# Gate weights held still, block means sent earlier, and the scale of 1/8 moved into the queries

## The chip, the cores and the metric

The kernel runs on one core of a Trainium2 chip. The metric is the device time of one execution in microseconds; several executions are timed and their median counts. A core has five engines with queues of their own: TensorE (PE in the profile, its weight loads PEld), VectorE (DVE), ScalarE (ACT), GpSimd (POOL) and SyncE (SP), which here only issues DMAs. They meet at semaphores.

## The reference, cut to what matters

Three stages follow one another: a banded attention with block summaries, then two mixture-of-experts layers. The change lies in the attention and in the router product that follows it.

```
# q, k, v: 4 batches, 8 heads, 768 rows, 64 columns
k_sum = k.reshape(B, H, 24, 32, D).max(axis=3)
v_sum = v.reshape(B, H, 24, 32, D).mean(axis=3)
scores_l = scale * q @ k.T, kept where |i - j| < 16, else -1e9      # scale = 1/8
scores_s = scale * q @ k_sum.T + log(32)
a = softmax over [scores_l, scores_s]
out = a @ [v, v_sum]                      # becomes x: 3072 tokens of 512
logits = x @ w_gate                       # 3072 x 8; tokens go to experts by these
```

## The kernel before

The attention works on units: a unit is one batch and one pair of heads, so that the 128 partitions hold 2 x 64 head columns. There are 16 units, four to a batch (`HP = 4`). A unit has 12 windows of 64 queries, and a window sees 96 keys and the 24 block summaries, 120 columns (`KW`). Four windows make a group (`GW = 4`), three groups a unit (`NG = 3`), 48 groups in all (`GROUPS`). Everything is in fp32 but the mask.

For a group `n`: `scores(n)` puts the mask and log(32) into a PSUM bank with one bf16 product (L1181) and adds four products of queries and keys (L1184). VectorE takes the maxima of the rows (`maxima`, L818 and L821), ScalarE the exponentials with their sums (`exps`, L652), VectorE the reciprocals (`recip`, L825 and L827), GpSimd multiplies (`normalize`, L472), TensorE transposes the probabilities (`probs_T`, L1193), VectorE copies them to SBUF (`evac_pT`, L833), TensorE multiplies them with the values (`times_v`, L1206, 16 passes), and ScalarE copies the output into `xT` (`evac_o`, L661).

The order on each engine is written out by hand as a loop over n. TensorE does in iteration n: `scores(n + 3)`, `times_v(n - 1)`, `probs_T(n)`, and, where n % 3 is 2, `logits` of the unit before (L1220). VectorE does `recip(n + 1)`, `maxima(n + 3)`, `evac_pT(n)`; where n % 3 is 0 also the maxima of the key blocks two units ahead (L791), where it is 2 a quarter of the value block sums of the next batch (`block_means`, L810, the last quarter also L813). ScalarE does `exps(n + 2)`, `evac_o(n - 1)`, and where n % 3 is 2 it issues the DMA that copies a unit's block means beside its value windows (`load_block_means`, L290, "vw<-vs" in the profile). That DMA waits for the means (`vs_ready`); `times_v` of a unit's first group waits for it. GpSimd does `normalize(n + 1)`, the key windows of a later unit (L458, L460; n % 3 is 0), its queries (L466, L467; n % 3 is 1), and constants for the later stages (n % 3 is 2; the longest block of them at n = 26). The queries of units 0 and 1 are spread by ScalarE (L666).

The router's logits are accumulated over the four units of a batch in one PSUM bank: six products per unit, one for each 128 tokens, with the tokens' columns of `xT` as the weights and the gate weights streamed, padded to 128 columns. VectorE copies a batch's 48 columns to `LM` (`logits_in`, L837). When the last batch's are there, VectorE starts the search that assigns tokens to experts.

The second layer's router has another form already (L1463): `wg2` with 32 columns as the weights, a tile of tokens streamed, and the three tiles of a phase written to partitions 0, 32 and 64 of one bank. ScalarE copies them out (L737) and a transpose turns them (L1467).

```
for c in range(KC):
    for j in range(CT):
        ins = mm(LP[32 * j:32 * j + 32, 0:128], wg2[:, c, :], yT[:, j, c, :], start=(c == 0), stop=(c == KC - 1))
```

Of the kernel before, what the change touches and what calls it, by code (L numbers as in the profile page):

```python
# [5 lines left out]
def banded_attention_two_moe_layers(nc, qT, kT, vwin, vblk, g1, w1a, w2a, skip2, g2, w1b, w2b, out):  # L6
    fp32, bf16, i32 = mybir.dt.float32, mybir.dt.bfloat16, mybir.dt.int32
    ALU = mybir.AluOpType
    ACT = mybir.ActivationFunctionType
# [16 lines left out]
    GW = 4  # L26
# [2 lines left out]
    NB = 3  # L29
    NP = 4  # L30
    SCALE = 1.0 / 8.0
    MASKED = -7985954816.0
    LOG_BLOCK = (27.75, -0.024169921875, 5.7220458984375e-05)
    NT = N // 128
    TB = S // 128
    KC = DM // 128
# [23 lines left out]
    with ctx:  # L60
        def sb(name, shape, dt=fp32):
            return ctx.enter_context(nc.sbuf_tensor(name, shape, dt))
# [19 lines left out]
        revE = sb("revE", [128, E])  # L82
        iotaS = sb("iotaS", [128, NSLOT])
        cnt128 = sb("cnt128", [128, NT])
        wg1 = sb("wg1", [128, KC, WIDE + E * (TB - 1)])
        wg2 = sb("wg2", [128, KC, 32])
        l2T = sb("l2T", [CT * 32, 128])

# [51 lines left out]
        def sba(name, shape, dt=fp32):  # L140
# [70 lines left out]
        bank = [ctx.enter_context(nc.psum_tensor(f"bank{i}", [128, 512], fp32)) for i in range(8)]  # L211

        SC, PT, OB, LG = bank[0:3], bank[3:5], bank[5:7], bank[7]
        LGP = LG[:, 0:TB * E]

        XB, HB, YB, SM, LP = bank[0:2], bank[2:4], bank[4:6], bank[6], bank[7]
        VTP, CNT, TAU = SM[:, 0:256], SM[:, 256:256 + WIDE], SM[:, 384:384 + WIDE]
# [5 lines left out]


        names = """q_in0 q_in1 q_in2 k_in0 k_in1 k_in2 v_in0 v_in1 v_in2 vb_in0 vb_in1 vb_in2 vb_in3 wg1_in const_in ident_ready zeros_ready pads_ready
            band_ready const_ready ksum_ready kw_ready kw_first qz_ready vb_sum vs_ready score_mm max_raw max_ready exp_done
            recip_ready norm_done sum_eps gaps_ready prob_tr prob_evac pv_done o_evac xr_tr xr_evac x_st0 x_st1 x_st2 x_st3
            logit_mm logit_in v_ready v_tr cnt_ready cnt_mm tau_diag tau_mm expert_ready expert_read rows_ready base_mm slot_ready
            onehot_ready blk_ready id_mm idp_ready ids_ready tok_c
            xg_in xg_tr xgT_ready w_in0 w_in1 w2_in0 w2_in1 h_mm h_act y_mm y_evac y_tr yT_ready l2_mm l2T_ready l2_tr l2_evac y_out y_st y_written  # L230
            gate_sub gate_exp rows8_ready base8_mm teA_ready onehot2_ready id2_mm gid2_ready route2_ready
# [62 lines left out]
        def own_part(spread_q, j):  # L294

            return spread_q[D * j:D * j + D, :, QW * j:QW * j + QW]

        def queries_of(q, j):

            return q[D * j:D * j + D, :].rearrange("d (w q) -> d w q", q=QW)  # L300
# [129 lines left out]
        def _(pool):  # L430
# [31 lines left out]
            def queries(u):  # L462
                i = u % NB
                pool.wait_ge(s[f"q_in{i}"], 16 * (u // NB + 1))
                pool.wait_ge(s["score_mm"], NG * (u - 1))
                o.step(g.tensor_copy(own_part(qz[u % 2], 0), queries_of(qc[i], 0)))  # L466
                g.tensor_copy(own_part(qz[u % 2], 1), queries_of(qc[i], 1)).then_inc(s["qz_ready"], 1)  # L467
                pool.wait_ge(s["qz_ready"], u + 1)

            def normalize(n):  # L470
# [169 lines left out]
        def _(act):  # L640
# [6 lines left out]
            def exps(n):  # L647
                act.wait_ge(s["max_ready"], n + 1)
                if n >= NP:
                    act.wait_ge(s["prob_tr"], n - NP + 1)  # L650
                for w in range(GW):
                    ins = a.activation(pr[:, n % NP, w, :], SC[n % 3][:, KW * w:KW * w + KW], ACT.Exp, scale=SCALE,  # L652
                                       bias=nmx[:, n % NP, w:w + 1], accum_out=rsum[:, n % NP, w:w + 1])
                ins.then_inc(s["exp_done"], 1)

            def evac_o(n):
                act.wait_ge(s["pv_done"], n + 1)
                u, gr = divmod(n, NG)
                b, hp = divmod(u, HP)
                at = S * b + GW * QW * gr  # L660
                a.activation(xT[:, hp, at:at + GW * QW], OB[n % 2][:, 0:GW * QW], ACT.Copy).then_inc(s["o_evac"], 1)  # L661

            for u in range(2):
                act.wait_ge(s[f"q_in{u}"], 16)
                for j in range(2):
                    ins = a.activation(own_part(qz[u], j), queries_of(qc[u], j), ACT.Copy)  # L666
                ins.then_inc(s["qz_ready"], 1)
                exps(u)
            for n in range(GROUPS):
                if n + 2 < GROUPS:  # L670
                    exps(n + 2)
                if n >= 1:
                    evac_o(n - 1)
                if n % NG == NG - 1 and 2 <= n // NG + 1 < U:
                    load_block_means(act, n // NG + 1)
            evac_o(GROUPS - 1)

            for t in range(NT):
                act.wait_ge(s["xr_tr"], t + 1)
# [93 lines left out]
        def _(dve):  # L773
# [40 lines left out]

            def maxima(n):
                dve.wait_ge(s["score_mm"], n + 1)
                raw = SC[n % 3][:, GW * KW:GW * KW + GW]
                ve.tensor_reduce(raw, SC[n % 3][:, 0:GW * KW].rearrange("p (w c) -> p w c", w=GW), X, ALU.max,  # L818
                                 negate=True).then_inc(s["max_raw"], 1)
                dve.wait_ge(s["max_raw"], n + 1)  # L820
                ve.tensor_scalar(nmx[:, n % NP, :], raw, SCALE, None, ALU.mult).then_inc(s["max_ready"], 1)  # L821

            def recip(n):
                dve.wait_ge(s["exp_done"], n + 1)
# [8 lines left out]
                ve.tensor_copy(pT[:, n % 2, :], PT[n % 2][0:KW, :]).then_inc(s["prob_evac"], 1)  # L833

            def logits_in(b):
                dve.wait_ge(s["logit_mm"], b + 1)
                ve.tensor_copy(LM[:, TB * b:TB * b + TB, :], LGP.rearrange("p (t e) -> p t e", e=E)) \  # L837
                    .then_inc(s["logit_in"], 1)

            ve.memset(wg1[:, :, :], 0.0)  # L840
            ve.memset(wg2[:, :, :], 0.0).then_inc(s["pads_ready"], 1)
# [11 lines left out]
            for n in range(GROUPS):  # L853
                if n + 1 < GROUPS:
                    recip(n + 1)
                if n + 3 < GROUPS:
                    maxima(n + 3)
                evac_pT(n)
                if n % NG == 0 and n // NG + 2 < U:
                    block_maxima(n // NG + 2)  # L860
                if n % NG == 2 and n // (NG * HP) + 1 < B:
                    block_means(n // (NG * HP) + 1, n // NG % HP)
                if n >= NG * HP and n % (NG * HP) == 2:
                    logits_in(n // (NG * HP) - 1)
            logits_in(B - 1)
            dve.wait_ge(s["logit_in"], B)
# [299 lines left out]
        def _(pe):  # L1166
# [43 lines left out]
            def logits(u):  # L1210
                b, hp = divmod(u, HP)
                if u == 0:
                    pe.wait_ge(s["wg1_in"], 16)
                pe.wait_ge(s["o_evac"], NG * (u + 1))
                if hp == 0 and b >= 1:
                    pe.wait_ge(s["logit_in"], b)
                for t in range(TB):
                    cover = hp == 0 and t == 0
                    wide = WIDE + E * (TB - 1) if cover else WIDE
                    ins = mm(LG[:, E * t:E * t + wide], xT[:, hp, S * b + 128 * t:S * b + 128 * t + 128], wg1[:, hp, 0:wide],  # L1220
                             start=cover, stop=(hp == HP - 1 and t == TB - 1))
                if hp == HP - 1:
                    ins.then_inc(s["logit_mm"], 1)

            def x_rows_tile(t):
                if t >= 2:
# [11 lines left out]
            for n in range(GROUPS):  # L1238
                if n + 3 < GROUPS:
                    scores(n + 3)  # L1240
                if n >= 1:
                    times_v(n - 1)
                probs_T(n)
                if n >= NG and n % NG == 2:
                    logits(n // NG - 1)
            times_v(GROUPS - 1)
            logits(U - 1)


            HID = KC * FC  # L1250
# [291 lines left out]
```

## Time and profile before

| | |
|---|---|
| median of 3 timed executions | 902.52 us (900.97 to 902.87) |
| the profiled execution | 897.85 us, its span 896.1 us |
| busy over the span | PE 849.3 us (95%), PEld 569.7 (64%), DVE 466.4 (52%), POOL 220.2 (25%), ACT 212.1 (24%) |
| the chain that ended last | PE 79%, DVE 13%, DMA 3%, issue 3%, POOL 2%, ACT 1% |
| TensorE's mean granted clock | 0.987 of full speed |

The span goes from the first instruction to the last. The shares are averages over stages of different kinds, so that they say little of one stage. The profiler's chain goes back from the last instruction, at each step to what released it. Matmuls are pipelined: a matmul's own duration holds its latency, and the distance between starts is what it costs in a row of them.

### The profile page before, as it was taken

Reading aid. Unit: us, or ns where it says so; the run is one execution under the profiler, and the core shown is the slowest. Engines: PE = TensorE matmul, PEld = TensorE weight load, DVE = VectorE, ACT = ScalarE, POOL = GpSimd, SP = SyncE. Lnnn points to the kernel's source line nnn. Section 1 sums busy time; section 2 is a strip of 40 time slices with the busy share of each in tenths; the row PEclk is TensorE's granted clock in tenths of the full one; section 3 lists DMA queues with packets and bytes.
Section 4 is the critical chain, followed back from the end, with each engine's and each line's share of the span. In section 5 each row is a group of like instructions: output and inputs, shape, how many; then the busy total and the mean of one; then the engine's idle time right before and its main releaser. Section 6 shows DMA issues by size and latency. Waiting matters only on the chain.

```text
span 896.1 us, 15627 instructions
## 1 busy us (share of the span) xinstructions
PE 849.3 (95%) x5212; PEld 569.7 (64%) x5212; DVE 466.4 (52%) x2118; ACT 212.1 (24%) x670; POOL 220.2 (25%) x321
## 2 busy tenths in 40 slices
PE   5899999798899999999999999999999999999997
PEld 4789888686345455454545555555777686777775
DVE  8689886677777676767677676070360000000000
ACT  4466565330102121221202121211111110101010
POOL 4678875001030110203021120203012121211111
PEclk8899999899999999999999999999999999999999
DMA  7987752345070523406071522555789988889880
GB/s 218 283 235 214 219 164 49 122 162 198 26 259 36 208 85 116 178 11 259 24 246 48 201 93 104 189 200 195 277 292 318 356 303 315 320 325 328 313 297 16
DMA packets 69271, 174.78 MB, mean 195 GB/s; under 512 B 6064, under 2 KB 10672, under 8 KB 69216
## 3 DMA queue, kind: packets, MB, share of 16 engines
q1 hardware_dynamic: 54600, 143.99, 46.8%
q0 software_dynamic: 6960, 21.69, 7.0%
q10 hardware_dynamic: 7656, 8.36, 2.8%
q8 instruction: 35, 0.57, 0.3%
q14 instruction: 20, 0.16, 0.1%
HBM read 149.19 MB, written 23.59 MB: 193 GB/s over the span
## 4 chain that ended last, share of the span: by engine, by line
PE 79%; DVE 13%; DMA 3%; issue 3%; POOL 2%; ACT 1%; DVEq 0%; POOLq 0%; SPq 0%; ACTq 0%
PE bank L1314 15%; PE bank L1300 15%; PE bank L1424 14%; PE bank L1435 14%; DVE junk L915 4%; PE bank L1184 4%; PE bank L1206 3%; PE bank L1193 3%; PE bank L1220 2%; PE bank L1373 2%; DMA vw<-vs 1%; PE bank L1289 1%; PE bank L1450 1%; PE bank L1413 1%; PE bank L1181 1%
## 5 line engine op out<-in xcount | busy, mean ns | idle before, releaser
L1300 PE MATMUL bank<-xgT,W 128*128 128x384 f32 x512 | 182.3, 497 | 0.6 <-ACT xgT L687 0.6
L1314 PE MATMUL bank<-W,hT 128*128 128x512 f32 x384 | 179.2, 602 | 0.0
L915 DVE TENSOR_SCALAR_CACHE_REDUCE junk<-Vt,cand 128x192 bf16<-128x192 f32 x376 | 136.1, 410 | 4.8
L1424 PEld LDWEIGHTS bank<-x2T,W 128*128 128x128 f32 x1152 | 131.4, 192 | 7.8 <-issue 7.8
L1424 PE MATMUL bank<-x2T,W 128*128 128x128 f32 x1152 | 131.9, 275 | 0.0
L1435 PE MATMUL bank<-W,h2T 128*128 128x512 f32 x288 | 126.7, 593 | 0.4 <-ACT h2T L754 0.4
L1072 DVE SCALAR_TENSOR_TENSOR o<-bank,gate,x 128x512 f32<-128x512 f32 x18 | 13.4, 751 | 211.6 <-PE bank L1435 211.6
L1300 PEld LDWEIGHTS bank<-xgT,W 128*128 128x128 f32 x512 | 89.6, 191 | 50.5 <-issue 5.7
L1314 PEld LDWEIGHTS bank<-W,hT 128*128 128x128 f32 x384 | 66.8, 190 | 58.4 <-issue 56.5
L1435 PEld LDWEIGHTS bank<-W,h2T 128*128 128x128 f32 x288 | 53.3, 190 | 60.9 <-issue 60.9
L652 ACT ACTIVATE pr<-bank,nmx 128x120 f32<-128x120 f32 x192 | 66.7, 363 | 33.5 <-DVE nmx L821 19.1
L754 ACT ACTIVATE h2T<-bank 128x512 f32<-128x512 f32 x36 | 21.4, 597 | 216.9 <-PE bank L1424 216.9
L692 ACT ACTIVATE hT<-bank 128x384 f32<-128x384 f32 x64 | 31.4, 490 | 141.5 <-PE bank L1300 141.5
L1184 PEld LDWEIGHTS bank<-kw,qz 128*128 128x128 f32 x384 | 55.9, 209 | 1.7
L1184 PE MATMUL bank<-kw,qz 128*128 128x120 f32 x384 | 55.4, 292 | 0.0
L472 POOL TENSOR_TENSOR pr<-pr,rinv 128x480 f32<-128x480 f32 x48 | 47.3, 985 | 30.5 <-DVE rinv L827 28.7
L281 POOL TENSOR_TENSOR hot_id<-hot,pnum 128x384 bf16<-128x384 f32 x7 | 8.2, 1167 | 179.6 <-DVE hot L979 179.6
L596 POOL COPY now_s<-sidx 128x1 int32 (+1 forms) x18 | 3.3, 183 | 193.3 <-DVE o L1072 193.3
L1373 PEld LDWEIGHTS bank<-cnt,same_e 128*128 128x128 bf16 x136 | 13.2, 97 | 57.8 <-DVE junk L915 54.3
L930 DVE TENSOR_SCALAR_CACHE_REDUCE reached<-bank 128x7 f32<-128x7 f32 x120 | 19.9, 166 | 54.2 <-PE bank L1373 54.2
L558 POOL DMA_INDIRECT xg<-x_rows,gidx x24 | 23.6, 984 | 90.6 <-DVE gidx L895 85.7
L565 POOL DMA_INDIRECT out<-yb,tok_i x24 | 23.6, 985 | 85.6 <-ACT yb L696 82.8
(265 smaller groups left out, 1046.1 us busy)
## 6 DMA issues: line engine op xcount, KB each, us to landing
W<-in_moe_w SPq DMA_DIRECT2D x52, 2048.0 KB, 9.0
vw<-in_vwin SPq DMA_DIRECT2D x16, 576.0 KB
qc<-in_qT SPq DMA_DIRECT2D x16, 384.0 KB, 6.5
kc<-in_kT SPq DMA_DIRECT2D x16, 384.0 KB, 7.9
vb<-in_vblk SPq DMA_DIRECT2D x16, 384.0 KB, 6.7
x_rows<-xr SPq DMA_DIRECT2D x24, 256.0 KB, 2.1
y_rows<-yb ACTq DMA_DIRECT2D x24, 256.0 KB, 2.0
vw<-vs ACTq DMA_DIRECT2D x14, 144.0 KB
```

The lines of the kernel that those rows point to most:

```text
L472: g.tensor_tensor(pr[:, n % NP, :, :], pr[:, n % NP, :, :], rinv[:, n % NP, :].unsqueeze(2).to_broadcast([128, GW, KW]), ALU.mult) \
L652: ins = a.activation(pr[:, n % NP, w, :], SC[n % 3][:, KW * w:KW * w + KW], ACT.Exp, scale=SCALE, bias=nmx[:, n % NP, w:w + 1], accum_out= ...
L692: a.activation(hT[:, r, :], HB[r % 2][:, 0:CAP], ACT.Relu).then_inc(s["h_act"], 1)
L915: ins = ve.tensor_scalar(junk[:, c, :], Vt[:, :], cand[:, c:c + 1].bitcast(fp32), 0.0, ALU.is_ge, ALU.add, accum_out=cnt[:, c:c + 1])
L1184: ins = mm(SC[n % 3][:, KW * w:KW * w + KW], qz[u % 2][:, GW * gr + w, :], kw[u % 2][:, GW * gr + w, :], start=False, stop=(w == GW - 1))
L1193: ins = tr(PT[n % 2][0:KW, 128 * w:128 * w + 128], pr[:, n % NP, w, :], ident[:, :])
L1206: ins = mm(OB[n % 2][D * j:D * j + D, QW * w:QW * w + QW], vw[i][:, GW * gr + w, D * j:D * j + D], pT[:, n % 2, 128 * w + QW * j:128 * w + ...
L1300: ins = mm(HB[r % 2][:, 0:CAP], w1[:, c, 128 * r:128 * r + 128], xgT[:, c, :], start=(c == 0), stop=(c == KC - 1))
L1314: ins = mm(YB[j % 2][:, :], hT[:, r, 128 * j:128 * j + 128], w2[:, r, :], start=(r == 0), stop=(r == FC - 1))
L1373: mm(CNT, same_e[:, :], cnt[:, :].unsqueeze(1).to_broadcast([128, WIDE // 8, 8]), start=True, stop=True).then_inc(s["cnt_mm"], 1)
L1424: ins = mm(HB2[h][:, 128 * c:128 * c + 128], W1[:, par, k * F + at:k * F + at + 128], x2T[par][:, k, :], start=(k == 0), stop=(k == KC - 1))
L1435: ins = mm(YB2[par][:, :], h2T[:, f, :], W2[:, par, f * DM:f * DM + DM], start=(f == 0), stop=(f == FC - 1))
```

## The change

- The logits are computed with the gate weights (32 columns, padded with zeros) as the stationary operand and 256 token columns streamed: three products per unit, to partitions 0, 32 and 64. They come out transposed. After a batch's last unit ScalarE copies 96 x 256 values to a new tile `lgT` (`evac_logits`, at n % 12 = 3 of the next batch), TensorE turns them with two transposes (`logit_rows`, n % 12 = 4), and VectorE copies them to `LM` (n % 12 = 4 instead of 2).
- The block means' DMA is issued at n % 3 = 0 instead of n % 3 = 2.
- The four quarters of the block sums are done at n = 2, 5, 7, 8 in the first batch and at n = 1, 2, 4, 7 of twelve in the others, instead of 2, 5, 8, 11.
- The factor 1/8 is applied as the queries are spread (GpSimd's copies become TENSOR_SCALAR; ScalarE's copies get a scale), and the mask and log(32) are stored times 1/8. So the exponential needs no scale, and the maxima are written once, negated, to `nmx`, which is its bias. L821 and the semaphore between the two are gone.

```
-    MASKED = -7985954816.0
-    LOG_BLOCK = (27.75, -0.024169921875, 5.7220458984375e-05)
+    MASKED = -7985954816.0 * SCALE
+    LOG_BLOCK = (27.75 * SCALE, -0.024169921875 * SCALE, 5.7220458984375e-05 * SCALE)
...
-        wg1 = sb("wg1", [128, KC, WIDE + E * (TB - 1)])
+        wg1 = sb("wg1", [128, KC, 32])
+        lgT = sb("lgT", [3 * 32, S // 3])
...
-        LGP = LG[:, 0:TB * E]
+        LGP = LG[:, S // 3:S // 3 + TB * 32]
...
-                o.step(g.tensor_copy(own_part(qz[u % 2], 0), queries_of(qc[i], 0)))
-                g.tensor_copy(own_part(qz[u % 2], 1), queries_of(qc[i], 1)).then_inc(s["qz_ready"], 1)
+                o.step(g.tensor_scalar(own_part(qz[u % 2], 0), queries_of(qc[i], 0), SCALE, None, ALU.mult))
+                g.tensor_scalar(own_part(qz[u % 2], 1), queries_of(qc[i], 1), SCALE, None, ALU.mult).then_inc(s["qz_ready"], 1)
...
-                    ins = a.activation(pr[:, n % NP, w, :], SC[n % 3][:, KW * w:KW * w + KW], ACT.Exp, scale=SCALE,
+                    ins = a.activation(pr[:, n % NP, w, :], SC[n % 3][:, KW * w:KW * w + KW], ACT.Exp,
...
+            def evac_logits(b):
+                act.wait_ge(s["logit_mm"], b + 1)
+                a.activation(lgT[:, :], LG[0:96, 0:S // 3], ACT.Copy).then_inc(s["lgT_ready"], 1)
...
-                if n % NG == NG - 1 and 2 <= n // NG + 1 < U:
+                if n >= NG * HP and n % (NG * HP) == 3:
+                    evac_logits(n // (NG * HP) - 1)
+                if n % NG == 0 and 2 <= n // NG + 1 < U:
                     load_block_means(act, n // NG + 1)
             evac_o(GROUPS - 1)
+            evac_logits(B - 1)
...
-                raw = SC[n % 3][:, GW * KW:GW * KW + GW]
-                ve.tensor_reduce(raw, SC[n % 3][:, 0:GW * KW].rearrange("p (w c) -> p w c", w=GW), X, ALU.max,
-                                 negate=True).then_inc(s["max_raw"], 1)
-                dve.wait_ge(s["max_raw"], n + 1)
-                ve.tensor_scalar(nmx[:, n % NP, :], raw, SCALE, None, ALU.mult).then_inc(s["max_ready"], 1)
+                ve.tensor_reduce(nmx[:, n % NP, :], SC[n % 3][:, 0:GW * KW].rearrange("p (w c) -> p w c", w=GW), X, ALU.max,
+                                 negate=True).then_inc(s["max_ready"], 1)
...
-                dve.wait_ge(s["logit_mm"], b + 1)
-                ve.tensor_copy(LM[:, TB * b:TB * b + TB, :], LGP.rearrange("p (t e) -> p t e", e=E)) \
-                    .then_inc(s["logit_in"], 1)
+                dve.wait_ge(s["logit_tr"], b + 1)
+                ve.tensor_copy(LM[:, TB * b:TB * b + TB, :].rearrange("p (k i) e -> p k i e", k=3),
+                               LGP.rearrange("p (i k e) -> p k i e", k=3, e=32)[:, :, :, 0:E]).then_inc(s["logit_in"], 1)
...
-                if n % NG == 2 and n // (NG * HP) + 1 < B:
-                    block_means(n // (NG * HP) + 1, n // NG % HP)
-                if n >= NG * HP and n % (NG * HP) == 2:
+                b, at = divmod(n, NG * HP)
+                when = (2, 5, 7, 8) if b == 0 else (1, 2, 4, 7)
+                if b + 1 < B and at in when:
+                    block_means(b + 1, when.index(at))
+                if n >= NG * HP and n % (NG * HP) == 4:
                     logits_in(n // (NG * HP) - 1)
...
-                for t in range(TB):
-                    cover = hp == 0 and t == 0
-                    wide = WIDE + E * (TB - 1) if cover else WIDE
-                    ins = mm(LG[:, E * t:E * t + wide], xT[:, hp, S * b + 128 * t:S * b + 128 * t + 128], wg1[:, hp, 0:wide],
-                             start=cover, stop=(hp == HP - 1 and t == TB - 1))
+                for k in range(3):
+                    at = S * b + S // 3 * k
+                    ins = mm(LG[32 * k:32 * k + 32, 0:S // 3], wg1[:, hp, :], xT[:, hp, at:at + S // 3],
+                             start=(hp == 0), stop=(hp == HP - 1))
...
+            def logit_rows(b):
+                pe.wait_ge(s["lgT_ready"], b + 1)
+                for i in range(TB // 3):
+                    ins = tr(LGP[:, 96 * i:96 * i + 96], lgT[:, 128 * i:128 * i + 128], ident[0:96, 0:96])
+                ins.then_inc(s["logit_tr"], 1)
...
+                if n >= NG * HP and n % (NG * HP) == 4:
+                    logit_rows(n // (NG * HP) - 1)
             times_v(GROUPS - 1)
             logits(U - 1)
+            logit_rows(B - 1)
```

## Rows read from the trace of the kernel before

**Rows 1.** The page's 40 slices, of which TensorE's, its clock's and the DMA's.
```profile
PE   5899999798899999999999999999999999999997
...
PEclk8899999899999999999999999999999999999999
DMA  7987752345070523406071522555789988889880
```

**Rows 2.** Timeline at the end of the attention stage.
```profile
159.19 1.60 PE L1220 MATMUL bank<-wg,xT 128*128 128x128 f32 x12 [0.48 <-ACT xT L661]
160.83 0.21 DVE L837 COPY LM<-bank 128x48 f32<-128x48 f32 x1 [3.35 <-PE bank L1220]
```

**Rows 3.** The chain that ended last, from 0 to 62 us: start, us, what.
```profile
37.49 6.82 DMA vw<-vs
...
46.71 0.61 PE bank L1206 x16
47.33 0.58 PE bank L1193 x4
47.91 1.34 PE bank L1220 x12
49.25 0.20 PE bank L1181
49.45 0.89 PE bank L1184 x8
```

**Rows 4.** Stretches: us; busy PE, PEld, DVE, ACT, POOL; PEclk, DMA share, GB/s.
```profile
20.00:40.00 20.00, 16.76 (x157) 15.07 (x157) 13.48 (x32) 9.78 (x51) 12.77 (x19) 0.75 0.98 269
67.50:75.70 8.20, 8.20 (x101) 7.58 (x100) 7.44 (x18) 5.38 (x27) 7.33 (x11) 1.00 0.77 233
75.70:83.90 8.20, 8.20 (x101) 7.58 (x101) 7.41 (x18) 5.38 (x27) 6.77 (x9) 1.00 0.80 229
```

**Rows 5.** Waits from 40 to 160 us: total us, times, longest.
```profile
PE bank L1206 <- DMA vw<-vs: 3.4, 4, 1.6
...
PE bank L1193 <- POOL pr L472: 1.1, 1, 1.1
...
...
PE bank L1206 <- DVE pT L833: 0.8, 1, 0.8
```

**Rows 6.** The chain from 330 to 336 us, the second router's product.
```profile
333.30 1.00 PE bank L1463 x24
```

**Rows 7.** Timeline from 58 to 62 us, ScalarE's DMA issue and who waited.
```profile
58.33 0.79 ACTq L290 DMA_DIRECT2D vw<-vs  x1
...
61.61 0.69 PE L1206 MATMUL bank<-pT,vw 120*64 120x64 f32 x16 [0.77 <-DMA vw<-vs]
```

**Rows 8.** Timeline from 87 to 89.3 us, VectorE and GpSimd.
```profile
87.21 0.64 DVE L818 TENSOR_REDUCE bank<-bank 128x4 f32<-128x480 f32 x1
...
87.88 0.16 DVE L821 TENSOR_SCALAR nmx<-bank 128x4 f32<-128x4 f32 x1
87.96 0.69 DVE L833 COPY pT<-bank 120x512 f32<-120x512 f32 x1
...
88.38 0.82 POOL L466 COPY qz<-qc 64x768 f32<-64x768 f32 x1
...
88.56 0.66 DVE L825 TENSOR_SCALAR rsum<-rsum 128x4 f32<-128x4 f32 x1
```

**Rows 9.** Groups of instructions, 0 to 185 us.
```profile
L472 POOL TENSOR_TENSOR pr<-pr,rinv 128x480 f32<-128x480 f32 x48 | 47.3, 985 | 30.5 <-DVE rinv L827 28.7 <-PE bank L1184 0.4
...
L810 DVE TENSOR_REDUCE vs<-vb 96x32 f32<-96x1024 f32 x16 | 19.2, 1204 | 1.2 <-DMA vb<-in_vblk 1.2
...
L661 ACT ACTIVATE xT<-bank 128x256 f32<-128x256 f32 x48 | 18.5, 385 | 32.3 <-PE bank L1206 32.2
...
L466 POOL COPY qz<-qc 64x768 f32<-64x768 f32 x14 | 11.4, 817 | 0.0
...
L506 POOL TENSOR_SCALAR iota_blk<-iota_blk 128x24 f32<-128x24 f32 x1 | 0.3, 288 | 0.1
```

More of the change, by code:

```diff
@@ L225, in banded_attention_two_moe_layers @@
         names = """q_in0 q_in1 q_in2 k_in0 k_in1 k_in2 v_in0 v_in1 v_in2 vb_in0 vb_in1 vb_in2 vb_in3 wg1_in const_in ident_ready zeros_ready pads_ready
-            band_ready const_ready ksum_ready kw_ready kw_first qz_ready vb_sum vs_ready score_mm max_raw max_ready exp_done
+            band_ready const_ready ksum_ready kw_ready kw_first qz_ready vb_sum vs_ready score_mm max_ready exp_done
             recip_ready norm_done sum_eps gaps_ready prob_tr prob_evac pv_done o_evac xr_tr xr_evac x_st0 x_st1 x_st2 x_st3
-            logit_mm logit_in v_ready v_tr cnt_ready cnt_mm tau_diag tau_mm expert_ready expert_read rows_ready base_mm slot_ready
+            logit_mm lgT_ready logit_tr logit_in v_ready v_tr cnt_ready cnt_mm tau_diag tau_mm expert_ready expert_read rows_ready base_mm slot_ready
             onehot_ready blk_ready id_mm idp_ready ids_ready tok_c
@@ L665, in _ @@
                 for j in range(2):
-                    ins = a.activation(own_part(qz[u], j), queries_of(qc[u], j), ACT.Copy)
+                    ins = a.activation(own_part(qz[u], j), queries_of(qc[u], j), ACT.Copy, scale=SCALE)
                 ins.then_inc(s["qz_ready"], 1)
```

## The prediction

> **What bounds the kernel now.** I read the page's 40 slices first [rows 1]: TensorE is busy for nine tenths and more from about 40 us on, at the full 2.4 GHz level in nearly every slice. The change touches only the attention stage. It ends at about 160.8 us, where VectorE copies the last logits [rows 2]; what follows is untouched, so I take a gain in the stage to be a gain in the total.
>
> The chain that ended last [rows 3] shows how the stage runs. A head pair (a unit) is three iterations of one group each, and a group costs TensorE 0.61 (L1206) + 0.58 (L1193) + 0.20 (L1181) + 0.89 (L1184) = 2.28 us, back to back. The third iteration has the logits block, 1.34 us (L1220). A unit is thus 3 x 2.28 + 1.34 = 8.2 us. The stretches of 8.20 us [rows 4] say the same: TensorE is busy in all of it, while VectorE has 7.4, GpSimd 6.8 to 7.3 and ScalarE 5.4 us of work. The waits from 40 to 160 us [rows 5] are few: four for the block means' DMA (3.4 us in all), one for GpSimd's normalize (1.1). The bound is TensorE's own work, with VectorE less than a microsecond per unit behind it. That nearness is the main risk.
>
> Before 40 us it is otherwise: a DMA share of 0.98 and half the clock in part of the stretch [rows 4].
>
> **Part by part, against the profiled execution's 897.85 us.**
>
> *Logits with gate weights stationary.* Before: 6 products per unit, each 128 token columns as weights and 128 columns streamed, 12 passes in 1.34 us. After: 3 products of 256 streamed columns against 32 weight columns, that is 6 passes. The streamed columns are the same 768, so if the passes ran one behind another nothing would be gained. But they write partitions 0, 32 and 64. The trace has this form already: the second router's L1463, also 32 weight columns on three partition offsets, does 24 passes of 128 columns in 1.00 us [rows 6]. L1220's rate is 1.34/12 = 0.112 a pass; 24 would take 2.68. So three run at once: 8 slots of 0.107 (0.86), with 0.14 left for getting in and out. A unit's new block is then 2 slots of 256 columns (2 x 0.213 = 0.43) + 0.14 = 0.57, rounded up to 0.58. Gain 0.76 us in each of the first 15 units: **-11.4**. Bounds: 0 if the passes don't overlap, -0.9 a unit if the 0.14 is not paid.
>
> A product in fp32 is two passes (12 for L1220's six products). Were these held in program order, tile 0's second pass would wait for its first, with tiles 1 and 2 queued behind, and a block would need 4 slots: 0.86 + 0.14 = 1.0, a gain of 0.34. L1463's 24 passes would then need 16 slots or more, 1.7 us; they took 1.00, so I leave this to a rival. The Trainium skill (TensorE: Matmul & The Clock Gate, Part 3) states that rule, matmuls in strict program order; by that rule alone the sum would be 6.3 us smaller, and the trace does not agree.
>
> *Rows of the logits (two transposes per batch).* L1193's transposes cost 0.58/4 = 0.145 each [rows 3], so 0.29 for a batch; three batches lie inside the stage: **+0.9**. ScalarE's copy of 96x256 is like its 128x256 copy L661, 0.39 us [rows 9], four times; it has 5.4 us of work in 8.2 [rows 4], so it is hidden.
>
> *The tail, fourth batch.* Before: from the block's start at 159.19 to VectorE's copy at 160.83 is 1.64 [rows 2]. After: block 0.43 and some 0.25 until the last result, ScalarE 0.4, two transposes with their latency 0.5: 1.6. **0**, bounds -0.2 to +0.5; the sixteenth unit's gain goes here.
>
> *Block means earlier.* Their DMA leaves ScalarE's queue at n%3==0 instead of n%3==2, two iterations sooner. At batch starts it had also to wait for the sums: issued at 58.33, and L1206 started at 61.61 after a wait of 0.77 for it [rows 7]. Now the sums of the next batch are done at n=8 (first batch) or n=7 of twelve, and the issue is at n=9. The time from issue to need becomes some 8 us (one unit of 7.4 + an iteration of 2.3 - 1.5 until ScalarE gets to it), against a worst landing of 6.8 [rows 3]. The four waits go: **-3.4**, bounds 0 to -3.4. Behind the issue on ScalarE stand the exponentials of group n+3, not needed for two iterations.
>
> *Maxima.* L821 falls out. It starts 0.08 before the pT copy, and the reduce now hands over without a wait, so VectorE gains about 0.19 us a group [rows 8], 0.5 a unit, and the exponentials start as much sooner. TensorE doesn't wait there, so no term by itself; it pays for the shorter unit. In the start-up chain, before TensorE saturates, I give it **-0.4** (bounds 0 to -1).
>
> *Block sums crowded (n = 1, 2, 4, 7 of twelve).* VectorE's unit becomes 7.4 - 0.5 = 6.9 us on average against TensorE's new 3 x 2.28 + 0.58 = 7.42. The unit that now has two sums (L810, 1.2 us each [rows 9]) has 8.1. Behind the pT copy TensorE has some 0.2 us of slack in a plain iteration and 0.8 in one with logits. Walking the order: the copies of n=2 to 5 come 0.1 to 0.5 late, then VectorE catches up at n=5 and 6. **+0.8** over three batches, bounds 0 to +4.5 (1.5 a batch). logits_in moves to n=4 and must be read before the block of n=5: just in time.
>
> *GpSimd scales the queries.* COPY of 64x768 takes 0.82 us [rows 8, 9]. TENSOR_SCALAR has one row there, 24 columns in 0.288, so its fixed part is not much over 0.26, while a second input costs 985/480 = 2.05 ns a column (L472). Bounds: 0.82 (as a copy) and 768 x 2.05 = 1.58. I take 0.95, nearest to the one-input rows. GpSimd's unit is then 6.8 + 0.3 = 7.1 of 7.42: hidden. One place isn't: at n=26 a block of constants already makes TensorE wait 1.1 [rows 5], and as the logits block of that iteration shrinks, the wait grows by it: **+0.8**. L825 also ran 0.66 instead of 0.16, ending as GpSimd's COPY L466 ended [rows 8]; a longer L466 stretches it by 0.1, inside the lag above.
>
> Sum: -11.4 + 0.9 + 0 - 3.4 - 0.4 + 0.8 + 0.8 = **-12.7**. On 897.85 that is 885.2. The three timed runs have a median of 902.52, 4.7 above the profiled one; I carry the difference over: **889.8 us**.
>
> **Rivals.**
> 1. *VectorE (or the DMA behind it) becomes the bound.* For: only 0.5 us between 6.9 and 7.42, the crowded sums, and a stretch with 0.77 DMA share at 8.2 us [rows 4] that needs 0.85 at 7.42. Against: the average still fits. With 1.5 us per batch lost and half of the four waits returning: -12.7 + 3.7 + 1.7 = -7.3, **895**.
> 2. *The passes keep program order*: 4 slots, 0.86 + 0.14 = 1.0, gain 0.34 a unit, 5.1 instead of 11.4: -6.4, **896**. Against it stands [rows 6].
> 3. *GpSimd's multiply runs at the two-input rate, and the kernel gets slower.* 2 x (1.58 - 0.82) = 1.5 more makes its unit 6.8 + 1.5 = 8.3 busy, and it idles up to 1 us per unit waiting for VectorE's reciprocals and block maxima. 8.85 instead of 8.21 for 14 units is +9.0, less 3.4: +5.6, **908**. It decides from 0.82 + (7.42 - 6.8)/2 = 1.1 us an instruction on, where the gain starts to go, and at 1.5 it is gone.
> 4. *The change doesn't do what it says*: no overlap of passes at all; 768 columns take 1.28 + 0.14, 0.08 more than now in 15 units. Then -12.7 + 11.4 + 1.2: -0.1, **902.4**.
> 5. *More comes*: the shorter chain before 40 us starts the saturated DMA earlier and saves a clock drop there: -16, **886.5**.
>
> **Chances.** Forecast (-10 to -15) 0.68; rival 1 0.13; rival 2 0.06; rival 3 0.05; rival 4 0.03; rival 5 0.05. Likeliest alone: 887.5 to 892.5. For 8 in 10 the range goes into rivals 1 and 5: 885.5 to 896.5. What this measurement can tell from no change is about 0.2%, 1.8 us. Faster 0.93, same 0.03, slower 0.04.
>
> **What would show it.** After: L1220's x6 at about 0.58 us until the next scores; units 7.4 to 7.5 us apart; no TensorE wait for vw<-vs after 40 us; GpSimd's query lines under 1.1 us; TensorE waiting on pT (L833's successor) only in the first half of a batch; the last LM copy near 148 us. I am wrong if the block takes 1.0 us, if query lines take 1.5, or if waits for pT or vw come in every unit.

## The result, and the profile after

The changed kernel is slower: a median of 924.91 us (924.06 to 927.58, 4 executions) against 901.83 us (900.97 to 902.87, 4 executions) before, a ratio of 1.026 with the interval 1.0234 to 1.0287. The forecast was 889.8 us, faster. The profiled execution took 925.70 us, its span is 923.4 us.

The page of the changed kernel, to be read against [rows 1]: TensorE's slices, its clock and the DMA share, then the chain's shares and two groups (busy us, mean ns, idle time before and who ended it).

```profile
PE   5788777879889999999999999999999999999997
PEclk9788989989999999999999999999999999999999
DMA  7976864134607061524325070727679889898880
...
PE 68%; DVE 13%; POOL 10%; issue 3%; DMA 3%; ACT 1%; SPq 1%; DVEq 0%; POOLq 0%; ACTq 0%
...
L473 POOL TENSOR_TENSOR pr<-pr,rinv 128x480 f32<-128x480 f32 x48 | 47.4, 987 | 19.3 <-DVE rinv L832 17.0
L1188 PE MATMUL bank<-band,spread 67*128 67x480 bf16 x48 | 20.2, 421 | 34.5 <-POOL qz L468 27.0
```

The end of the attention stage is the last copy of the logits, the counterpart of [rows 2], in the timeline:

```profile
187.22 0.21 DVE L842 COPY LM<-bank 128x48 f32<-128x48 f32 x1 [2.77 <-PE bank L1234]
```

The stage ends at 187.2 instead of 160.8, 26.4 us later; the spans differ by 27.3. So the loss is in the stage. GpSimd's share of the chain has gone from 2% to 10%, and the first score product of an iteration idles 34.5 us, 27.0 of them ended by the spread queries (qz). TensorE's waits from 40 to 180 us (total, times, longest) put it in one row; the block means' DMA of [rows 5] is gone from it:

```profile
PE bank L1188 <- POOL qz L468: 25.5, 13, 3.1
PE bank L1200 <- POOL pr L473: 2.6, 1, 2.6
PE bank L1213 <- DVE pT L838: 0.2, 1, 0.2
```

Thirteen units, thirteen waits. The groups on GpSimd in the same stretch name the instruction; [rows 9] has COPY at 817 ns here:

```profile
L468 POOL TENSOR_SCALAR qz<-qc 64x768 f32<-64x768 f32 x12 | 25.5, 2128 | 1.0
L467 POOL TENSOR_SCALAR qz<-qc 64x768 f32<-64x768 f32 x12 | 25.5, 2125 | 0.0
```

The prediction named query lines of 1.5 us as a sign that it would be wrong. The timeline from 101.9 to 106.6 us shows how the instruction comes to the path:

```profile
101.97 2.12 POOL L467 TENSOR_SCALAR qz<-qc 64x768 f32<-64x768 f32 x1
...
103.48 0.63 PE L1226 MATMUL bank<-xT,wg 128*32 128x256 f32 x6
...
104.17 2.13 POOL L468 TENSOR_SCALAR qz<-qc 64x768 f32<-64x768 f32 x1
...
106.36 0.38 PE L1188 MATMUL bank<-band,spread 67*128 67x480 bf16 x1 [2.24 <-POOL qz L468]
...
106.38 0.99 POOL L473 TENSOR_TENSOR pr<-pr,rinv 128x480 f32<-128x480 f32 x1
```

TensorE has done its logits block by 104.1 and stands until the second multiply ends at 106.30. GpSimd goes on at once with the next normalize. This repeats every 9.84 us where nothing else disturbs a unit. Two stretches of one unit each tell who sets the pace (us, busy PE, PEld, DVE, ACT, POOL, clock, DMA share, GB/s):

```profile
77.00:86.80 9.80, 8.72 (x88) 7.24 (x88) 7.24 (x15) 5.67 (x28) 7.69 (x7) 0.78 0.74 193
96.50:106.30 9.80, 7.60 (x93) 6.34 (x93) 6.12 (x13) 5.42 (x28) 9.41 (x9) 1.00 0.77 200
```

At full clock GpSimd is busy 9.41 of 9.80 us and TensorE 7.60; in [rows 4] it was 7.3 at most against 8.20. The first stretch shows a second, smaller price: beside such waits TensorE's granted clock fell to the 1.2 GHz level for a while (6.8 us from 74.5 on; the mean of the stretch is 0.78).

### The profile page after: what moved, and what is told of

The parts are those of the page before. It is cut to its first block, busy times and chain, and to the rows that moved or that the text cites. A ratio compares the mean times of both kernels' runs of the same rounds, so it can differ in the third digit from the quotient of the medians.

```text
span 923.4 us, 15407 instructions
## 1 busy us (share of the span) xinstructions
PE 849.8 (92%) x5124; PEld 558.6 (60%) x5124; DVE 460.9 (50%) x2070; ACT 214.6 (23%) x674; POOL 257.4 (28%) x321
## 4 chain that ended last, share of the span: by engine, by line
PE 68%; DVE 13%; POOL 10%; issue 3%; DMA 3%; ACT 1%; SPq 1%; DVEq 0%; POOLq 0%; ACTq 0%
PE bank L1315 15%; PE bank L1329 14%; PE bank L1439 14%; PE bank L1450 13%; DVE junk L922 4%; POOL qz L467 3%; POOL qz L468 3%; POOL pr L473 2%; PE bank L1191 2%; PE bank L1388 1%; DMA kc<-in_kT 1%; PE bank L1213 1%; PE bank L1200 1%; DVE ks L799 1%; PE bank L1304 1%
## 5 line engine op out<-in xcount | busy, mean ns | idle before, releaser
L700 ACT ACTIVATE hT<-bank 128x384 f32<-128x384 f32 x64 | 31.4, 491 | 141.4 <-PE bank L1315 141.4
L1191 PEld LDWEIGHTS bank<-kw,qz 128*128 128x128 f32 x384 | 60.9, 226 | 1.8
L1191 PE MATMUL bank<-kw,qz 128*128 128x120 f32 x384 | 60.3, 309 | 0.0
L1188 PE MATMUL bank<-band,spread 67*128 67x480 bf16 x48 | 20.2, 421 | 34.5 <-POOL qz L468 27.0
```

The lines of the kernel that those rows point to most:

```text
L700: a.activation(hT[:, r, :], HB[r % 2][:, 0:CAP], ACT.Relu).then_inc(s["h_act"], 1)
L1191: ins = mm(SC[n % 3][:, KW * w:KW * w + KW], qz[u % 2][:, GW * gr + w, :], kw[u % 2][:, GW * gr + w, :], start=False, stop=(w == GW - 1))
```

## The experiments

The change has four parts: the logits streams, the earlier block means, the scale moved into the queries (with the one-step maxima), and GpSimd's multiply inside it. The first runs undo or do one part each. My theory at that point: the multiply on GpSimd is the whole loss. The rival: the shorter unit exposes some other wait, so that the kernel would stay slow without the multiply.

**The scale part alone, on the kernel before.** The queries are multiplied by 1/8 on GpSimd and ScalarE, the exponential loses its scale, the maxima are one step; logits and block means as before.

> The kernel before with the scale part alone: GpSimd multiplies the queries by 1/8, no second step of the maxima. Theory G (GpSimd's multiply is the whole loss): its two instructions take 2.13 us each as in the changed kernel, GpSimd has 3 x 0.99 + 2 x 2.13 + 1.14 + 0.43 + 0.94 = 9.7 us per unit against 8.2, and the time is that of the changed kernel, 922 to 928. Theory S (the streams or the crowded sums cost too, GpSimd only a part): clearly less, 908 to 916.

Measured: 923.92 against 902.96 us, ratio 1.0236 (1.0209 to 1.0263). Its groups on GpSimd, and its waits from 40 to 180 us:

```profile
L467 POOL TENSOR_SCALAR qz<-qc 64x768 f32<-64x768 f32 x14 | 29.9, 2135 | 1.2
...
PE bank L1178 <- POOL qz L467: 18.1, 13, 2.3
```

The undisturbed units are 9.84 to 9.88 us apart, as in the changed kernel (9.84), though the logits block here is the old, longer one. With GpSimd as the bound, what TensorE saves is not seen.

**The changed kernel without the scale part.**

```
-                o.step(g.tensor_scalar(own_part(qz[u % 2], 0), queries_of(qc[i], 0), SCALE, None, ALU.mult))
+                o.step(g.tensor_copy(own_part(qz[u % 2], 0), queries_of(qc[i], 0)))
```

The same for the other half; the exponential has its scale again and the maxima their second step.

> The changed kernel with the scale part undone: GpSimd copies the queries as before (0.82 us), the maxima have their second step again, streams and block means stay changed. G: the gain that was forecast for the rest appears, less 0.19 us a group on VectorE: 889 to 894, units 7.4 to 7.7 us apart. S: 902 or more.

Measured: 893.47 against 902.96 us, ratio 0.9894 (0.9866 to 0.9922). The rest of the change is worth 9.5 us. The chain of this kernel in one unit, beside [rows 3]:

```profile
71.10 0.20 PE bank L1191
71.31 0.89 PE bank L1194 x8
72.19 0.61 PE bank L1216 x16
72.81 0.58 PE bank L1203 x4
73.39 0.56 PE bank L1229 x6
73.95 0.31 PE bank L1191
```

The block takes 0.56 us where it took 1.34. The score product behind it takes 0.31 instead of 0.20, which I had not counted. The undisturbed units are 7.53 to 7.54 us apart; where a wait falls into one it takes up to 11.8. From the first logits block to the fifteenth it is 112.9 us here and 145.9 in the changed kernel.

**The changed kernel with the queries on ScalarE.** ScalarE spreads and multiplies the queries of all units, as it did for the first two; GpSimd's two instructions fall out.

```
+                if n % NG == 1 and n // NG + 2 < U:
+                    queries(n // NG + 2)
...
+                for j in range(2):
+                    ins = a.activation(own_part(qz[u % 2], j), queries_of(qc[i], j), ACT.Copy, scale=SCALE)
```

> The changed kernel, but ScalarE spreads and scales the queries of all units (two ACTIVATE of 64x768, 0.84 us each, at n % 3 = 1), GpSimd none. G: GpSimd falls to 5.3 us a unit, ScalarE rises from 5.4 to 7.1 of 7.42: 887 to 892. If ScalarE's queue of evacuations and exponentials then comes late for TensorE: 894 to 900, with TensorE waiting for xT or VectorE for the exponentials. S: 902 or more.

Measured: 893.58 against 902.96 us, 0.9904 (0.9875 to 0.9933), between the two expected ranges and as fast as the run with copies. The multiply costs nothing that can be measured where an engine has room for it.

**The logits part alone, on the kernel before.** Products, their copy and transposes as changed; sums, block means and scale as before. It was to give the block's gain by itself.

> The kernel before with the logits part alone: gate weights held still, three products of 256 columns per unit, two transposes per batch. G: the block falls from 1.34 to about 0.6 us, 15 units, less 0.9 for the transposes and up to 1 for VectorE's lag: 891 to 894. S or a hidden cost of the streams: 898 or more.

Measured: 915.62 against 902.96 us, ratio 1.0135 (1.0101 to 1.0169): slower, and I had not seen it coming. So there is a second effect, of some 22 us against the run without the scale part, from which it differs by the block means' times alone. Its waits from 40 to 180 us, and its chain from 60 to 70 us:

```profile
PE bank L1214 <- DMA vw<-vs: 19.7, 6, 4.8
```

```profile
60.79 1.13 DVE vs L818
...
61.94 0.23 DVE vs L821
...
62.20 6.64 DMA vw<-vs
...
68.89 1.13 PE bank L1214 x16
```

and the timeline, where SyncE's next loads begin:

```profile
62.20 0.79 ACTq L291 DMA_DIRECT2D vw<-vs  x1
62.40 0.33 SPq L325 DMA_DIRECT2D vw<-in_vwin  x1
```

The sums end at 62.17, the issue is at 62.20, and 0.2 us later SyncE begins the next unit's burst of loads, 1.7 MB. The 144 KB copy takes 6.64 us to be seen. In the kernel before, the issue at 58.33 [rows 7] was 0.9 us ahead of the burst (59.21). At the other two batch starts the lead is 0.9 us before (92.2, 126.8) and 0.2 to 0.3 us here (104.2, 142.0). From issue to the end of the last packet the three copies took 2.6, 2.6 and 2.5 us before, and 5.7, 5.4 and 5.1 here. The lead is not all, though: the copy issued here at 89.72, 2.9 us ahead of its burst, took 6.2, and TensorE waited 2.77 us for it. Around the stalls the clock falls too (3.4 or 6.8 us at half, from 67.7, 98.4, 108.7 and 146.2 on). This was a reading of traces; the next runs were made to test it.

**The block means part alone, on the kernel before**: the sums at n = 2, 5, 7, 8 and then 1, 2, 4, 7 of twelve, the issue at n%3==0.

> The kernel before with the block means part alone (sums earlier, DMA two iterations earlier), L1220's block of 1.34 us kept. My forecast for the part: the four waits go, 3.4 us, 898 to 900. Rival: the DMA now falls into SyncE's burst and takes 6 to 11 us, but it is wanted 8.9 us after its issue, so nothing or up to 1 us is gained: 901 to 903.

Measured: 901.01 against 903.88 us, 0.9956 (0.9932 to 0.998), a gain of 4.0 us by the ratio (1.8 to 6.1). The forecast's term was 3.4. By its median alone the run falls into the rival's range, and the rival's mechanism is there too: a unit's copy is now issued 0.07 us behind the burst, as long as there are bursts, and then takes 4.7 to 7.2 us from 60 us on. It is wanted late enough: TensorE waits for it once after 40 us (1.9). Alone the part is small; beside the logits part it is some 22 us.

**The logits part with the earlier sums, the issue still at n%3==2.**

```
-                if n % NG == 2 and n // (NG * HP) + 1 < B:
-                    block_means(n // (NG * HP) + 1, n // NG % HP)
+                b, at = divmod(n, NG * HP)
+                when = (2, 5, 7, 8) if b == 0 else (1, 2, 4, 7)
+                if b + 1 < B and at in when:
+                    block_means(b + 1, when.index(at))
```

> The run with the logits part alone was slower than the kernel before, with TensorE waiting 19.7 us for vw<-vs; the one at batch starts left ScalarE 0.2 us before SyncE's burst of input loads and took 6.6 us, where before the change it left 0.9 us ahead and took 2.5. This kernel is that one with the block sums at n = 1, 2, 4, 7, the issue still at n % 3 = 2. Theory D (the means' DMA falls into the burst because the sums come late): the issue no longer waits for the sums and leaves 2 us or more before the burst, 2.5 to 4 us each, waits for vw<-vs under 3 us, 889 to 894. Theory E (it is the two iterations that the issue was moved by that cured it): still over 905.

Measured: 900.95 against 903.88 us, 0.9961 (0.9941 to 0.9982); 8.6 us of waits in five instead of 19.7. The sums alone bring most of it (from 1.0135 to 0.9961), the earlier issue the rest (to 0.9894). Neither expectation was met in full: the late sums count, and some waits stay without them.

**The logits part with SyncE's loads held back**: the burst that begins with a unit waits until that unit's block means have landed (`v_in` counts the value windows and the means), so that it no longer stands beside their copy.

```
+                if u > NB:
+                    sp.wait_ge(s[f"v_in{(u - 2) % NB}"], 32 * ((u - 2) // NB + 1))
```

> The kernel before with the logits part alone (the run that waited 19.7 us for vw<-vs), and one more wait on SyncE: the burst of a unit's input loads starts only when the block means that ScalarE has issued for the unit then beginning have landed. Nothing else differs. D: the means' DMA again takes 2.4 to 3 us, also at batch starts, TensorE's waits for it fall from 19.7 to 3 to 6 us, and 898 to 903 result. E: no change or slower, 913 or more.

Measured: 905.97 against 902.81 us, 1.0021 (0.999 to 1.0051). Against the logits part alone, some 1.1% come back with the sums as late as ever, so that the burst has a share. But TensorE waits 19.2 us as before, now in eleven pieces (longest 3.4). Four pieces of the chain show why:

```profile
61.16 4.15 DMA vw<-vs
...
87.29 7.66 DMA vw<-vs
...
100.69 5.27 DMA vw<-vs
...
138.87 2.82 DMA vw<-vs
```

At the three batch starts (61.16, 100.69, 138.87) the copy is seen after 4.15, 5.27 and 2.82 us, where it was 6.64, 6.47 and 5.71 without the hold. In the other units a held burst begins late, and the next copy meets it: the one issued at 87.29 left 3.1 us behind a burst and took 7.66. So the hold shortens the stalls at batch starts and makes new ones elsewhere. Both expectations missed: only one of the three copies took the 2.4 to 3 us that were forecast.

**The logits part with a lighter load.** The value blocks of batches 2 and 3 are loaded in 2 of their 32 columns; the rest of that load is left out, so its total is not comparable with any other.

> The kernel before with the logits part alone, but of batches 2 and 3 each quarter of the value blocks loads 2 columns instead of 32, so that their block sums are made of what the buffer held (that part of the work is left out; the last LM copy, not the total, is to be compared). This takes some 370 KB from each unit's 1.87 MB from the fifth unit on. Theory D2 (the input loads nearly fill the DMA engines at 7.5 us a unit, and the means' DMA waits behind them): its waits after 80 us, 11 to 12 us in that run, fall under 4 and the last LM copy comes at 165 to 170 instead of 178.6. If the late sums alone place the DMA badly, whatever the load: 10 us or more of waits stay, LM copy after 174.

Measured: the last logits copy at 172.07 (178.59 with the full load); waits of 4.76 us at 104.99 and 4.23 at 142.01 stay. The one at 97.01 (2.77 us), which is not at a batch start, is gone. After 80 us 10.1 us of waits are left, as the second theory had it; the last copy lies between the two forecasts. This load is thus only a part: the burst's other loads, window values, queries and keys, stay at their place just behind the issue. Only the late sums put the issue there, since in the other units nothing holds it.

**The means two units ahead**, once on the changed kernel without the scale part, once on the one with the queries on ScalarE, with one edit for both:

```
-                if n % NG == 0 and 2 <= n // NG + 1 < U:
-                    load_block_means(act, n // NG + 1)
+                if n % NG == NG - 1 and n // NG + 2 < U:
+                    load_block_means(act, n // NG + 2)
```

> The changed kernel with the scale part undone, and the means' DMA at n % 3 = 2 two units ahead, in the lull before SyncE's burst. D: it takes 2.5 to 4 us each instead of up to 11, is ready a unit before it is wanted, and TensorE's 3.1 us of waits for vw<-vs after 40 us go, with one clock drop: 887 to 891. If the waits were for the windows themselves (the larger load on the same semaphore): no change, 892 to 895.

> Streams, earlier sums, ScalarE spreading and scaling the queries, no second step of the maxima, and the means' DMA at n % 3 = 2 two units ahead. D: waits for vw<-vs after 40 us under 2 us, otherwise like the run with ScalarE spreading: 887 to 892. If the saturated stretch before 60 us sets the waits whatever the order: 892 to 896.

Measured: 895.23 us, 0.9891 (0.986 to 0.9922), no difference to the same kernel without it, and its waits for the means are 5.1 us, not gone as the first theory had it; and 891.57 against 902.81 us, **0.9875** (0.9858 to 0.9891), the fastest kernel of the study, faster than both. It beats the other ScalarE version by less than the two intervals can tell. Its waits from 40 to 180 us and its end of the stage:

```profile
PE bank L1221 <- DMA vw<-vs: 2.3, 2, 1.7
PE bank L1208 <- POOL pr L473: 2.2, 2, 2.0
```

```profile
152.38 0.21 DVE L850 COPY LM<-bank 128x48 f32<-128x48 f32 x1 [2.77 <-PE bank L1242]
```

**GpSimd's multiply as a product with a constant tile**: in the changed kernel, TENSOR_TENSOR with a small tile that holds 1/8 (12 columns, each read 64 times).

> The changed kernel with GpSimd's multiply as a TENSOR_TENSOR with a constant tile. G: 985/480 = 2.05 ns a column give 1.6 us an instruction instead of 2.13; GpSimd's unit falls from 9.8 to 8.7 us, still the bound: 14 units save 15 us, 907 to 912. If the instruction costs the same 2.1 us: 922 or more.

Measured: 909.88 us in its one execution, the instruction at 1466 and 1470 ns, waits for it of 9.6 us in 11. The product with this second input is faster than the multiply by a number: 1.47 against 2.13 us. So "two inputs" does not explain 2.13, and I measured the instruction by itself.

**The instruction by itself**: in the kernel with the queries on ScalarE, GpSimd runs ten kinds on a spare tile behind its constants, each three times.

> The kernel with ScalarE spreading the queries, and after the attention stage, where GpSimd is idle, ten GpSimd instructions on a spare tile, three times each: copy and multiply of 64x768 with the queries' spread pattern, multiply of 64x768 and 128x768 without it, of 128x384 and 128x96, add and multiply-add of 128x768, a TENSOR_TENSOR and a copy of 128x768. G says that TENSOR_SCALAR costs per column: 2.1, 2.1, 2.1, 1.1 and 0.4 us for the five multiplies. If the spread pattern or the 64 partitions make it slow: 2.1 us for the first alone, 0.9 for 128x768 without it. If arithmetic of any kind is slow on GpSimd, the TENSOR_TENSOR takes as long as the TENSOR_SCALAR.

The groups of this run on GpSimd:

```profile
L583 POOL TENSOR_SCALAR scr<-scr 128x768 f32<-128x768 f32 x3 | 6.4, 2139 | 0.2
L586 POOL TENSOR_SCALAR scr<-scr 128x768 f32<-128x768 f32 x3 | 6.4, 2136 | 0.2
L581 POOL TENSOR_SCALAR scr<-scr 64x768 f32<-64x768 f32 x3 | 6.4, 2133 | 0.3
L582 POOL TENSOR_SCALAR scr<-scr 64x768 f32<-64x768 f32 x3 | 6.4, 2123 | 0.2
L588 POOL TENSOR_TENSOR scr<-scr 128x768 f32<-128x768 f32 x3 | 5.4, 1810 | 0.2
L584 POOL TENSOR_SCALAR scr<-scr 128x384 f32<-128x384 f32 x3 | 3.6, 1190 | 0.2
L587 POOL TENSOR_SCALAR scr<-scr 128x768 f32<-128x768 f32 x3 | 2.5, 832 | 0.2
L589 POOL COPY scr<-scr 128x768 f32<-128x768 f32 x3 | 2.5, 822 | 0.2
...
L585 POOL TENSOR_SCALAR scr<-scr 128x96 f32<-128x96 f32 x3 | 1.3, 448 | 0.2
```

L583 multiplies, L586 adds, L581 writes into spread places, L582 plainly: all 2.12 to 2.14 us, on 64 partitions or 128. So it is neither the operation nor the layout. Nor does the work beside it show: VectorE was busy for 0.69 of 2.10 us beside one of them (149.2) and for 1.70 of 2.20 beside another (153.6). It grows by (2139 - 448) / (768 - 96) = 2.5 ns a column. L587 is the same instruction with two operations, multiply and add, and takes 0.83 us like a copy. A TENSOR_TENSOR with a full second tile takes 1.81 (L588).

**The changed kernel with the multiply written in that form**, nothing else:

```
-                o.step(g.tensor_scalar(own_part(qz[u % 2], 0), queries_of(qc[i], 0), SCALE, None, ALU.mult))
+                o.step(g.tensor_scalar(own_part(qz[u % 2], 0), queries_of(qc[i], 0), SCALE, 0.0, ALU.mult, ALU.add))
```

> The changed kernel with one thing different: GpSimd's multiply by 1/8 is written as multiply and add 0.0, since the multiply-add of 128x768 took 0.83 us where the multiply alone took 2.13. Theory G (the slow single-operation form is the whole loss): the instructions take 0.83 us, GpSimd's unit is 6.9 us again, and the time is that of the run with the scale part undone or a little less, 888 to 893. If the zero that is added costs as the single form: 922 or more.

Measured: 896.62 against 903.81 us, ratio 0.9922 (0.9893 to 0.995). Its query group, and its waits from 40 to 180 us:

```profile
L468 POOL TENSOR_SCALAR qz<-qc 64x768 f32<-64x768 f32 x14 | 11.7, 833 | 1.2
```

```profile
PE bank L1213 <- DMA vw<-vs: 5.2, 3, 2.4
...
PE bank L1200 <- POOL pr L473: 3.0, 2, 2.1
...
PE bank L1188 <- POOL qz L468: 0.9, 2, 0.5
```

One operand and one operation more in two source lines turn +2.6% into -0.8%. That settles the cause of the loss. The forecast of 888 to 893 was missed by some 3 us: the run is near the one with copies (0.9894), their intervals overlap, and the waits for the means are 5.2 us here against 3.1 there.

**The same form with the scale part alone, and with the means two units ahead:**

> The kernel before with the scale part alone, the multiply written with two operations. Theory G: the loss of 21 us of the one-operation form is gone; TensorE stays the bound at 8.2 us a unit and the freed 0.5 us of VectorE buys at most 1 us: 900 to 903. If the new order on VectorE or the scaled band costs anything by itself: 905 or more.

> The same, and the means' DMA at n % 3 = 2 two units ahead, as in the fastest run so far (ratio 0.9875). 886 to 891; like that run or better, since ScalarE has its 1.7 us per unit back. If the saturated stretch sets the time: 891 to 894.

Measured: 905.55 against 903.81 us, 1.0011 (0.9985 to 1.0038), and 897.69 us, 0.9931 (0.9908 to 0.9953). The scale part in its cheap form is worth nothing that can be told from zero. The means two units ahead bring nothing here, and the 886 to 891 expected of them was missed; in the profiled execution a wait of 4.28 us for them stands at 62.12, behind the stretch before 60 us in which the DMA engines are full (a share of 1.03 from 40 to 57 us in the fastest kernel, 0.91 in the kernel before).

## Why the prediction was wrong

The step that failed is the last term, *GpSimd scales the queries*: 0.95 us an instruction, bounds 0.82 to 1.58. It measured 2.13, outside both bounds. The mechanism was written down as rival 3 with its condition ("at 1.5 it is gone") and given 0.05. With the measured price, its own working comes out: 2 x (2.13 - 0.82) = 2.6 more makes GpSimd's unit 6.8 + 2.6 = 9.4 busy (9.41 in the stretch above), and 0.4 of idle (it had allowed up to 1) gives 9.84. Against 7.53 without the scale part that is 2.3 in each of 14 units, 32 us; the medians, of different sessions, differ by 31.4 (924.91 and 893.47). Units with other waits are longer in both, but the stretch over all of them differs by 33.1 (145.9 and 112.9).

Two choices made the term too small. I took the value nearest to a row with an instruction of 24 columns [rows 9], 288 ns, that tells nothing of the slope: 448 ns at 96 columns (measured afterwards) would have. And I closed the range above with the two-input rate, as if a multiply by a number could not be slower than a product of two tiles; it is (2.13 against 1.47 on the same shape, and 1.81 with a full second tile). Where the deciding instruction has no row of its size, a chance of 0.05 for the side that decides was not held by anything.

The other terms, by their steps:

- *Logits with gate weights stationary*, -11.4: right in mechanism, a little too large. The block is 0.56 for 0.58 forecast, and three products on different partition offsets ran together, as [rows 6] said. (The working for passes in program order counts 16 slots for L1463; with neighbours of different tiles together, as in its own 4 slots a block, 13 are enough, 1.4 us. The 1.00 measured rules that out all the same.) But the first score product behind it grew by 0.11. The unit fell from 8.21 to 7.53, not 7.42: 0.68 x 15 = 10.2 us.
- *Rows of the logits*, +0.9: two transposes are 0.17 in the chain, then the first score product. The unit with them is 7.70 against 7.53 where nothing else is waited for, 0.17 for 0.29: right in kind, a little too large.
- *The tail*, 0: from the last block's start to VectorE's copy 1.54 us (154.35 to 155.89) where it was 1.64. Right.
- *Block means earlier*, -3.4: alone -4.0 by the ratio, right in size. The worst landing in it was not: the copies issued at 42.02 and 91.17 in the run without the scale part took 10.2 and 9.4 us to their last packet, where the working had 6.8 at worst against some 8 of room. What I also missed is that the part is a condition for the streams. I had counted four waits on the DMA that would go, and not asked what happens to them when the unit gets 0.68 shorter while VectorE, which makes the sums, doesn't. Without the part the kernel is 1.35% slower than before, with it 1.06% faster (both without the scale part).
- *Maxima* -0.4, *constants at n=26* +0.8: in the fastest kernel the wait for the normalize was 2.0 us at 100.23, where [rows 5] had 1.1: 0.9 for 0.8. GpSimd has no queries there, so this fits but does not prove the term. The maxima can't be told from zero (1.0011, 0.9985 to 1.0038).
- *Block sums crowded*, +0.8: the waits for the pT copy after 40 us are 1.2 us in three in the run without the scale part, 0.8 in one before [rows 5]: 0.4. Within its bounds.
- The sum without the scale part's terms was -12.7 + 0.4 - 0.8 = -13.1, and measured is -9.5 (the interval of the ratio, 0.9866 to 0.9922, is -12.1 to -7.0). The block accounts for 1.2 of the difference. Waits for the means stay too, 3.1 us in three after 40 us, where I had none; those I had put into rival 1. That 893.47 lies inside the range of 885.5 to 896.5 says little for the forecast, which was for the whole change.

What stays open: which transfer delays the means in the full stretch before 60 us, and why their waits move from one kernel to the next (a single wait of 7.63 us stood at 48.81 in the scale part alone in its cheap form, 1.1 us of them in all after 40 us in the longer form). The stall at batch starts is shown to depend on when the sums are done, and the run with the loads held back moved the burst alone: the copies there became faster (6.64, 6.47, 5.71 to 4.15, 5.27, 2.82 us), so the burst has a share. That its 0.2 us of distance is the whole reason is not shown, and two of the three copies were slow without it. Which of the older transfers slowed them was not tested.

## What to carry to other kernels

An instruction that the trace doesn't show at its size, on an engine that has under a microsecond of room per unit, is to be bounded by its own slope or not at all; a neighbour of another kind is no upper end. Where a number decides the sign and nothing measured holds it, its bad side deserves more than a chance of 0.05. And when a change shortens a loop, list what is paced by another engine (here VectorE's sums in front of a DMA): it keeps its place in time and comes late in the new loop, so that two parts that seem separate are worth nothing, or less, one without the other.

## What the runs showed of the hardware

- GpSimd's TENSOR_SCALAR with one operation takes 2.5 ns a column in fp32: 448, 1190 and 2139 ns for 96, 384 and 768 columns, whether it multiplies or adds. With two operations, multiply and add, 768 columns take 832 ns; COPY takes 822, TENSOR_TENSOR 1810 with a full second tile and 1470 with a small one that is read repeatedly. I had expected the form with less to do to be at least as fast.
- The 144 KB copy of the block means took 2.5 us from issue to its last packet with nothing beside it, and 4.6 to 12.3 us where SyncE's loads began within 0.3 us of its issue. With the loads 2.9 us behind it (the logits part alone) it took 2.5 to 6.2.
- A stall of TensorE can cost more than its length. In the logits part alone the stalls of 2.8 to 4.9 us from 60 us on each had 3.4 or 6.8 us at half the clock that began inside them or within 1.5 us of their end. It is not so for every stall: with the loads held back, one of 3.18 us that ended at 94.99 was followed by full clock until 107.0.
- Three fp32 products on partitions 0, 32 and 64, of 256 columns and two passes each, took 0.56 us together, against 1.34 for 12 passes of 128 columns on full weights.
